# A mixed recurrence, routing and expert kernel on one core: fillers in TensorE's waits, setup constants in the last chunk, and a tile's rows sent to memory by SyncE

## What is computed

```python
# 1: a gated recurrence per batch and head, over t
m_new = max(f_gate[t] + m, i_gate[t])
C = exp(f_gate[t] + m - m_new) * C + exp(i_gate[t] - m_new) * outer(v[t], k[t])
n = exp(f_gate[t] + m - m_new) * n + exp(i_gate[t] - m_new) * k[t]
y[t] = sigmoid(o_gate[t]) * (C @ q[t]) / max(abs(n @ q[t]), 1)
# 2: routing: (token, expert) pairs in falling order of x @ w_gate; a token goes
#    to the first expert that still has room (384 places each)
h = relu(x[mask_e] @ w1[e]);  out[mask_e] = h @ w2[e]          # 320 -> 1024 -> 320
# 3: one more layer pair for all tokens
h = x @ w_in;  g = max(h, 0) + alpha * min(h, 0);  out = g @ w_out   # 320 -> 2048 -> 320
```

## Time and profile before

| | |
|---|---|
| median of 3 runs | 785.16 us (784.6 to 786.09) |
| the profiled execution | 785.32 us, span 783.2 us |
| TensorE products busy | 734.6 us (94%), 5911 instructions |
| VectorE busy | 571.9 us (73%) |
| ScalarE busy | 322.7 us (41%) |
| GpSimd busy | 153.8 us (20%) |
| chain that ended last | PE 85%, DVE 6%, issue 3%, ACT 2%, DMA 1% |

### The profile page before, as it was taken

How to read it: one execution, slowest core, us unless ns; L and a number is a source line. 1 busy time by engine, 2 the same in 40 slices (tenths; PEclk the granted TensorE clock), 3 DMA queues, 4 the chain that set the end, 5 groups by cost and what they waited for, 6 DMA issues and landing times.

```text
span 783.2 us, 17825 instructions
## 1 busy us (share of the span) xinstructions
PE 734.6 (94%) x5911; PEld 689.5 (88%) x5911; DVE 571.9 (73%) x1458; ACT 322.7 (41%) x775; POOL 153.8 (20%) x246
## 2 busy tenths in 40 slices
PE   5999999853999999999999999999999999999994
PEld 4899999742989988998999899889989998999994
DVE  7778888977677868776877778677868777783442
ACT  5666777302234513532361245134413522361431
POOL 6367787401000110110011001101100110011001
PEclk9999999955899999999999999999999999999998
DMA  6888886104104100500320041005001400410000
GB/s 160 251 227 237 224 229 179 42 12 138 42 1 149 31 26 4 175 26 0 88 90 25 0 147 30 25 0 163 31 9 52 125 25 0 142 36 25 1 1 26
DMA packets 66781, 62.54 MB, mean 80 GB/s; under 512 B 35004, under 2 KB 57916, under 8 KB 66748
## 3 DMA queue, kind: packets, MB, share of 16 engines
q1 hardware_dynamic: 57016, 48.66, 21.8%
q0 software_dynamic: 2688, 8.65, 3.5%
q10 hardware_dynamic: 7044, 4.79, 2.0%
HBM read 53.43 MB, written 8.65 MB: 79 GB/s over the span
## 4 chain that ended last, share of the span: by engine, by line
PE 85%; DVE 6%; issue 3%; ACT 2%; DMA 1%; ACTq 1%; POOL 0%; SPq 0%; DVEq 0%
PE bank L924 21%; PE bank L930 18%; PE bank L929 18%; PE bank L948 5%; PE bank L949 4%; PE bank L800 4%; PE bank L783 2%; PE bank L751 2%; PE bank L734 2%; PE bank L974 1%; PE bank L839 1%; PE bank L973 1%; ACT decay L1079 1%; PE bank L848 1%; PE bank L918 1%
## 5 line engine op out<-in xcount | busy, mean ns | idle before, releaser
L924 PE MATMUL bank<-wo_hi,h_hi 128*128 128x320 f32 x384 | 120.6, 314 | 0.0
L930 PE MATMUL bank<-wo_hi,h_lo 128*128 128x320 f32 x384 | 118.6, 309 | 0.0
L929 PE MATMUL bank<-wo_lo,h_hi 128*128 128x320 f32 x384 | 118.0, 307 | 0.0
L1627 DVE SCALAR_TENSOR_TENSOR g_act<-g_neg,rest_alpha,bank 128x384 f32<-128x384 f32 x128 | 78.4, 613 | 40.2 <-ACT g_neg L1161 38.1
L658 POOL DMA_INDIRECT xe<-x_rows,idx_in x24 | 27.0, 1127 | 398.8 <-DVE idx_in L1565 357.7
L1161 ACT ACTIVATE g_neg<-bank 128x384 f32<-128x384 f32 x128 | 62.6, 489 | 94.9 <-PE bank L949 94.9
L1165 ACT CAST h_hi<-g_act 128x384 fp32r<-128x384 f32 x128 | 65.8, 514 | 83.7 <-DVE g_act L1627 83.2
L1159 ACT ACTIVATE h_hi<-bank 128x384 fp32r<-128x384 f32 x64 | 31.5, 492 | 162.3 <-PE bank L949 157.0
L924 PE MATMUL bank<-yT_hi,wi_hi 128*128 128x384 f32 x256 | 92.1, 360 | 0.0
L1632 DVE TENSOR_TENSOR h_lo<-g_act,h_hi 128x384 fp32r<-128x384 f32 x128 | 71.2, 556 | 26.2 <-ACT h_hi L1165 22.5
L929 PE MATMUL bank<-yT_lo,wi_hi 128*128 128x384 f32 x240 | 81.3, 339 | 0.0
(11 more groups left out here) (247 smaller groups left out, 1740.5 us busy)
## 6 DMA issues: line engine op xcount, KB each, us to landing
s<-w SPq DMA_DIRECT2D x8, 1024.0 KB, 5.2
s<-w SPq DMA_DIRECT2D x16, 480.0 KB, 7.2
s<-w SPq DMA_DIRECT2D x16, 256.0 KB, 6.0
k_in<-kT SPq DMA_DIRECT2D x48, 80.0 KB
q_in<-qT SPq DMA_DIRECT2D x48, 80.0 KB
k_row<-k SPq DMA_DIRECT2D x24, 160.0 KB, 3.4
v_in<-v SPq DMA_DIRECT2D x24, 160.0 KB, 3.9
gate_o<-o SPq DMA_DIRECT2D x24, 160.0 KB, 3.3
```

What stands on the lines that cost most here:

```text
L924: pe.matmul(acc, ah, bh, start=start, stop=False, skip_group_check=True)
L929: pe.matmul(acc, ah, bl, start=False, stop=False, skip_group_check=True)
L930: return pe.matmul(acc, al, bh, start=False, stop=stop, skip_group_check=True)
L1627: dve.scalar_tensor_tensor(out=g_act[:, n, :], in0=g_neg[:, :], scalar=rest_alpha[:, j:j + 1], in1=acc, op0=ALU.mult, op1=ALU.add).then_in ...
```

## The change

- `x_sb` and the semaphores `x_out` become four, one for each batch. SyncE writes the rows (`send_rows`): those of tile T - 4 right after it has started `gate_o` of tile T, those of the last four after its last load. VectorE waits also for `x_turned` before it writes a buffer.
- `keep_busy(n, dst)` puts n products of the identity with itself, whose result nobody reads, on TensorE: 14 before the first gates, 5, 2 and 2 in the tail of attention, 12, 3 and 3 before the transposes of the first rows, 2 after them.
- ScalarE's decay waits for `bias_ready`, counted after the first of the three gate copies, not for all three.
- `routing_consts` and `search_consts` move from chunk 0 to chunk 5; `route_tie` counts in `consts`, and VectorE waits for it in `early_bests`.
- `split_peak(1)` runs after the probs of tile 1, not before them.
- w1 comes in slices with a semaphore each (`stage1_in[t]`), and each cast waits for its own; for the first expert ScalarE does `activate(0, 0)` before the second cast of w2.
- In `up`, the first product of the third slice waits for the high part only. In the last `down1` the search's product `add_four` stands one product earlier.

```diff
-        x_sb = ga("x_sb", [P, 2, DM])
+        x_sb = ga("x_sb", [P, B, DM])
...
+            def send_rows(c, b):
+                sp.dma_start(x_rows_by_tile[c, b][:, 0:DM], x_sb[:, b, :]).then_inc(x_out[b], 16)
+                sp.dma_start(x_rows_by_tile[c, b][:, DM:3 * P], x_sb[:, b, 2 * P:DM]).then_inc(x_out[b], 16)
...
                 sp.dma_start(gate_o[:, b, :], o[T]).then_inc(o_in[b], 16)
+                if not first(T, B):
+                    send_rows(c - 1, b)
...
-                sp.dma_start(s1[:, 0:2, :], w1[w, 0:2 * P, :].rearrange("(t p) f -> p t f", p=P)).then_inc(stage1_in, 16)
...
+                for t in range(2):
+                    sp.dma_start(s1[:, t, :], w1[w, P * t:P * t + P, :]).then_inc(stage1_in[t], 16)
...
+            def keep_busy(n, dst):
+
+                for _ in range(n):
+                    pe.matmul(dst[:, 0:P], ident[:, :], ident[:, :], start=True, stop=True)
+
+            keep_busy(14, XTB)
             turn_gates(0)
...
                 if isinstance(T, int) and T >= NT:
+                    keep_busy(5 if T == NT else 2, SCORE[0])
                     pe.wait_ge(out_read, NT)
                     pe.wait_ge(logit_read, T - 2)
                     router(*prev(c, b, 2))
+                if isinstance(T, int) and T == NT:
+                    keep_busy(2, SCORE[0])
...
+                keep_busy(12, UP[2])
                 for m in range(CT):
+                    if m:
+                        keep_busy(3, UP[2])
                     pe.wait_ge(first_rows[m], 16)
...
                 if ready:
+                    pe.wait_ge(ready if highs is None else highs, count + 3)
+                pe.matmul(acc, wh[:, 2, js], ah[:, 2, :], start=False, stop=False, skip_group_check=True)
+                if highs is not None:
                     pe.wait_ge(ready, count + 3)
                 if ready is y_ready:
                     pe.wait_ge(y_twice, count // 3 + 1)
-                pe.matmul(acc, wh[:, 2, js], ah[:, 2, :], start=False, stop=False, skip_group_check=True)
...
                 if b == 0:
-                    act.wait_ge(gates_ready, c + 1)
+                    act.wait_ge(bias_ready, c + 1)
...
-                act.dma_start(x_rows_by_tile[c, b][:, 0:DM], x_sb[:, b % 2, :]).then_inc(x_out[b % 2], 16)
-                act.dma_start(x_rows_by_tile[c, b][:, DM:3 * P], x_sb[:, b % 2, 2 * P:DM]).then_inc(x_out[b % 2], 16)
...
             high_w2(0, 0)
+            activate(0, 0)
             high_w2(0, 1)
-            activate(0, 0)
...
-                if not first(T, 2):
-                    dve.wait_ge(x_out[n], 32 * (c * (B // 2) + b // 2))
+                if not first(T, B):
+                    dve.wait_ge(x_out[b], 32 * c)
+                    dve.wait_ge(x_turned, T - B + 1)
```

More of the change, by code:

```diff
@@ L281, in build_program @@
         gates_ready = sem("gates_ready")
+        bias_ready = sem("bias_ready")
         qk_in = [sem(f"qk_in{b}") for b in range(B)]
@@ L293, in build_program @@
         state_ready = sem("state_ready")
-        x_out = [sem(f"x_out{n}") for n in range(2)]
+        x_out = [sem(f"x_out{b}") for b in range(B)]
         y_done = sem("y_done")
@@ L322, in build_program @@
         token_sum = sem("token_sum")
-        stage1_in = sem("stage1_in")
+        stage1_in = [sem(f"stage1_in{t}") for t in range(3)]
         stage2_in = [sem(f"stage2_in{t}") for t in range(3)]
@@ L483, in _ @@
                 load_tile(NCH - 1, b)
+            for b in range(B):
+                sp.wait_ge(x_ready, NT - B + b + 1)
+                send_rows(NCH - 1, b)
             sp.wait_ge(y_done, NT)
-            for n in range(2):
-                sp.wait_ge(x_out[n], 32 * NT // 2)
+            for b in range(B):
+                sp.wait_ge(x_out[b], 32 * NCH)
             sp.wait_ge(logit_done, NT)
@@ L631, in _ @@
             pool.sem_inc(prep_lo, 4)
-            weigh_values(0, 0)
-            routing_consts()
-            weigh_values(0, 1)
-            search_consts()
-            weigh_values(0, 2)
-            weigh_values(0, 3)
+            for b in range(B):
+                weigh_values(0, b)
             weigh_values(1, 0)
@@ L645, in _ @@
                 if b == 1:
+                    search_consts()
+                if b == 2:
                     mask_consts()
+            routing_consts()
             list_consts()
@@ L675, in _ @@
             pool.sem_inc(out_free, 1)
-            for n in range(2):
-                pool.wait_ge(x_out[n], 32 * NT // 2)
+            for b in range(B):
+                pool.wait_ge(x_out[b], 32 * NCH)
             fetch_rows(0)
@@ L831, in _ @@
             over_chunks(pe, step, tail=(0, 1))
-            pe.wait_ge(consts, 5)
+            pe.wait_ge(consts, 7)
             def count(ph, n):
@@ L919, in turn_rows, with parts3 @@
                 ins.then_inc(xe_turned, 1)
-            def parts3(acc, a, b, start, stop, low=None):
+            def parts3(acc, a, b, start, stop, low=None, between=None):
                 (ah, al), (bh, bl) = a, b
@@ L929, in parts3 @@
                 pe.matmul(acc, ah, bl, start=False, stop=False, skip_group_check=True)
+                if between:
+                    add_four(*between)
                 return pe.matmul(acc, al, bh, start=False, stop=stop, skip_group_check=True)
@@ L970, in down1 @@
                             ins = parts3(ACC[t][:, 0:CAP], (w2_hi[:, j, ds], w2_lo[:, j, ds]),
-                                         (h_hi[:, j % 3, :], h_lo[:, j % 3, :]), j == 0, j == J1 - 1)
+                                         (h_hi[:, j % 3, :], h_lo[:, j % 3, :]), j == 0, j == J1 - 1,
+                                         between=(ph, J1 - 2) if route and j == J1 - 1 and t == 0 else None)
                         else:
@@ L977, in down1 @@
                             ins.then_inc(y_acc, 1)
-                        if route and j == J1 - 1 and t == 0:
-                            add_four(ph, J1 - 2)
                     if route and j == J1 - 1:
@@ L1035, in _ @@
             turn_first()
+            keep_busy(2, UP[2])
             pe.wait_ge(prep_lo, 3 * PREP + 4)
@@ L1254, in copy_gates @@
                     ins = dve.tensor_copy(dst[:, cs, :].rearrange("p c h -> p (c h)"), GATES[i][:, 0:n])
+                    if i == 0:
+                        ins.then_inc(bias_ready, len(GROUPS[g]))
                 ins.then_inc(gates_ready, len(GROUPS[g]))
@@ L1351, in early_bests @@
                 ch = early
+                dve.wait_ge(consts, 7)
                 ch.link(dve.tensor_reduce(row_ones[:, :], ident[:, :].rearrange("p (c r) -> p r c", r=QR), X, ALU.add))
@@ L1412, in make_x @@
                 ch.link(dve.tensor_tensor(scaled[:, :, :], hsum[:, :, 0:D], bc(rnorm[:, :], D), ALU.mult))
-                if not first(T, 2):
-                    dve.wait_ge(x_out[n], 32 * (c * (B // 2) + b // 2))
+                if not first(T, B):
+                    dve.wait_ge(x_out[b], 32 * c)
+                    dve.wait_ge(x_turned, T - B + 1)
                 dve.wait_ge(tanh_ready, T + 1)
-                dve.scalar_tensor_tensor(out=x_sb[:, n, :], in0=gate_o[:, b, :], scalar=1.0, in1=scaled[:, :, :].rearrange("p h d -> p (h d)"),
+                dve.scalar_tensor_tensor(out=x_sb[:, b, :], in0=gate_o[:, b, :], scalar=1.0, in1=scaled[:, :, :].rearrange("p h d -> p (h d)"),
                                          op0=ALU.add, op1=ALU.mult).then_inc(x_ready, 1)
@@ L1424, in step @@
                 if first(T, B):
+                    if b == 0:
+                        split_peak(1)
                     if b == 2:
@@ L1587, in _ @@
             match_rows(ch, 0)
-            dve.wait_ge(consts, 7)
+            dve.wait_ge(consts, 8)
             own_list(ch, 0)
```

14 lines of the change are left out of this document (6 added, 8 removed).

## The result

The changed kernel takes **786.88 us** (785.02 to 788.3) beside 785.16 for the kernel before, run on the same chip: a ratio of 1.0021, 95% interval 1.0013 to 1.0029. It is slower by about 1.7 us; the forecast was 3.6 us faster. The profiled execution took 786.99 us (span 785.2) against 785.32, so it can be read for the difference: +1.67.

A forecast was written before the change was run, and what follows sets the result against it. TensorE was taken as nearly full in attention and experts, with soft places at the start, routing search and first expert's loads. -1.9 + 0.2 + 0 - 0.5 - 1.4 = -3.6 from 785.3 gave 781.7 us; own range 779.5 to 783.6, stated 779.3 to 787.0.

The forecast's parts named there:

- part 2: Attention loop: row writes on SyncE relieve ScalarE, -1.1 us; SyncE's debt costs about 0.2; bounds with the start -3.0, +3.4.
- rival (a): Attention loop: SyncE becomes the bound, 787 to 790 us, chance 0.12; partly bound, near 785.5, another 0.12.
- p = 6.5: SyncE's us a tile in the loop from which the kernel was said to get slower; over 0.2% slower from 6.6.
- p = 6.4: SyncE's us a tile in the loop, between early and later pace; time given as 785.3 + 0.2 = 785.5 us.
- Part 1: First 26 us: fillers raise TensorE's clock, decay waits for the bias first, peak split later; -1.0 us, bounds 0.4 to 1.5.
- Part 3: Last attention chunk: GpSimd's constants moved there collide with VectorE's key chain; +0.2 us, bounds 0 and +1.0.
- Part 4: End of attention: nine fillers in TensorE's waits may hold the clock a few us past 155.75, but VectorE covers it; 0.
- Part 5: Handover to the first expert: earlier casts by slice semaphores, fillers raise the clock; -0.5 us, bounds -1.1 and +0.8.
- Part 6: Hidden-to-output turn of each expert: first product waits for the high part only; 0.17 us eight times, -1.4, bounds -1.8 and -0.6.

The follow-up runs named there:

- k9: Changed kernel with rows issued by ScalarE, with the old start: no fillers before the gates, decay after all three copies, peak split before the second tile; 781.61 us, 0.9953.
- k13: Changed kernel, row writes kept on SyncE, k and q loaded together with two starts a tile in place of four; 780.57 us, 0.9927 of the kernel before.
- k14: Changed kernel with k and q loaded together (two starts in place of four) and the row writes back on ScalarE; 781.47 us, 0.9943 of the kernel before.
- k3: Changed kernel with rows issued by ScalarE and both groups of GpSimd's constants back in chunk 0; 781.08 us, 0.9951 of the kernel before.
- k6: Changed kernel with rows issued by ScalarE, without any of the fillers; 783.4 us, 0.997 of the kernel before.
- k12: Changed kernel with rows issued by ScalarE, one semaphore for all of w1, first activation behind the second cast, fillers kept; 781.81 us, 0.9957 of the kernel before.

## Why the prediction was wrong, by its own steps

**The step that failed is the price of SyncE's tile in part 2, and the slack it was set against.** The price was read off one tile: 4.96 us without waiting, 5.06 with the branch, and 1.1 for the row writes, 6.16 together. The twelve late tiles took 6.43 on average. That one tile was of the kind with wi_raw and wo_raw; every second tile has the two rest_raw starts, which take 0.57 and 0.53 us, not 0.41 and 0.41. Without their row writes the late tiles of the changed kernel take 5.0 us in the first kind and 5.45 in the second. The row writes take 1.12 in a tile like that at 99.81, but in four of the twelve the first of them takes 0.59 to 0.80 instead of 0.36, so they cost 1.2 on average. The four early tiles took 6.98, not 6.6, and the loop began 0.5 us later than the 19.47 counted from.

From there the working of the prediction gives the result: the loads of tile 20 start at 125.08, not 119.8, of which 0.5 lie at the start of the loop, 1.5 in the early tiles and 3.3 in the late ones. The scores start 4.53 later at 129.61 (4.5 was taken), 3.45 after where they stood. This is a sum that fits, not one wait: the trace has the last wait for q at tile 19 (loads 118.81, scores 123.77), and the scores of tile 20 only follow behind it. The other parts bring 1.8 (1.7 was taken), and +3.45 - 1.8 is the +1.67 measured. The 5.3 us between forecast and result are the 5.3 us by which those loads are late.

The prediction had this case twice: as the upper bound of part 2 (+3.4, loads at 125.1, landed at 129.6) and as rival (a), SyncE the bound, at 0.12. It put both wrongly below the forecast. The rival's deciding figure p = 6.5 agrees with the runs (6.57 measured, just slower; 6.02, no loss; 7.39, far slower). Its time for p = 6.4 has a slip: by its own formula that is 0.2 less the 1.7 of the other parts, 783.8 and not 785.5. That 786.9 still lies below the 787.0 at which the stated range ends is no merit of the forecast.

What misled was in the rows. The argument for the low price was that SyncE waits about 1 us a tile late in the loop. Added up, its waits in the kernel before are 9.5 us up to the loads of tile 20, 0.8 for each of the twelve late tiles and none in the four early ones; the other 10.4 us of its waits for x and for TensorE come behind those loads, too late to help. The change adds 1.1 to each of the 16, some 18 us. That alone puts the loads of tile 20 at 113.54 + 18 - 9.5 = 122, an estimate from these numbers, and the forecast of 119.8 out of reach. A second tile would not have shown it: the pair from 77.52 to 89.92 takes 12.40 us with 2.3 of waits, 5.05 a tile, since the start of gate_o takes 0.36 us behind a wait and about 0.5 where SyncE goes straight on.

The Trainium skill ("DMA: Bandwidth & Descriptors", section "Issuing engines are not separate DMA queues") says that transfers started from several engines share the 16 DMA engines and that what is saved is the sequencer's time to start them. The runs agree with it: with the same bytes the kernel takes 781.5 from ScalarE, 786.9 from SyncE and 792.4 from GpSimd, by how full the list of each is; of the last, 4.3 us stand behind the last output copy and have no known cause.

**Part 1, the start: right.** 1.06 at the first value product for 1.0. The fillers took 5.60 us and ended at 8.31 (8.4 was taken), scores took 1.16, VectorE's first probs came at 11.40 (11.35). The experiments don't confirm it in the median (k9). The clock's times in the prediction are a little off: in finer stretches of the kernel before it falls at 155.5, not 155.75, and is back at about 199.88, not 199.56, so 4.6 us after 195.32 and not 4.3.

**Part 2, ScalarE's side: about half.** 0.5 us by the traces of k13 and k14, where 1.1 was taken; TensorE's idle time did go to zero in k13, but part of it goes with the rows on ScalarE too.

**Part 3, the constants: right in the mechanism, small in the sum.** Three operations were longer by 0.3 each, more than one half collision of 0.2, and x of the last tile came 0.6 later against the last value product. Against that the prediction counted no gain for the first chunk, where k3 shows 0.85; the medians show nothing. The Trainium skill ("SBUF — State Buffer", section "Who interferes with whom") says that some VectorE operations, tensor_scalar among them, can take ports that are shared with GpSimd, and that whoever comes first keeps them to the end of its instruction. The three ends 0.1 us behind GpSimd's agree.

**Part 4, the fillers in the tail: right.** The last logits were read at 162.77, 3.93 later, as x of the last tile was. The granted clock stayed at its upper level until about 164.4, where it fell at 155.5 before, and no time came of it.

**Part 5, the first weights: right in kind, small by half.** 1.1 us in place of 0.5. The casts begin at 190.73, 192.26 and 194.51, the first of them 3.7 us earlier against the rest of the program, and the transposes of the rows took 0.55, not 0.90, so the clock had risen before them. The first product came only 0.4 earlier against x of the last tile (+3.56 for +3.93); the rest of the gain lay in the rounds after it, now at full clock. From x of the last tile to the first product of hidden to output it is 45.25 us before, 44.08 in the changed kernel, 44.07 in its twin with the rows on ScalarE, 45.37 without fillers (k6) and 44.78 without the slices (k12). So the gain of 1.2 is gone without the fillers, and over half of it without the slices: the two need each other and can't be added up.

**Part 6, the turns: right.** 1.23 over seven turns, 0.176 each, for 0.17. The two rows that answer to the earlier trace rows:

```profile
372.65 0.34 PE L972 MATMUL bank<-yT_hi,wi_hi 128*128 128x384 f32 x1
373.07 0.44 PE L977 MATMUL bank<-yT_lo,wi_mix 128*128 128x384 f32 x1
```

The high-part product now runs on without a gap, and the wait stands before the low-part one.

## What to carry to other kernels

A queue of transfers is an engine with a pace of its own: before starts are moved to it, add up all that one period of the loop costs it, over every kind of iteration, and set that beside the period of the bound engine. Count a queue's waits as slack only up to the transfer that decides, here 9.5 us against 18 us of added starts. When it is too full, make starts fewer, not smaller: 2 KB starts cost 0.8 to 1.0 us each here, while joining k and q in memory gave back all the time that the moved rows had cost.

## What the runs showed of the hardware

- What a start costs the queue did not follow its size: 160 KB of k_row 0.36 us, a row write of 32 KB 0.35, v_in with 8 pieces a row 0.59, and 2 KB from memory to memory 0.8 to 1.0. From one start to the next it was mostly 0.1 to 0.35 more. Single starts of the same kind sometimes took twice as long or more (k_row 1.62 at tile 6, the first row write 0.80 at tile 13); what delays them is not shown.
- One start of k and q together took about what one of k alone took (two in 0.83 to 0.87 us, against 0.83 to 0.95 for two of k), with twice the bytes.
- The one program with plain row writes in GpSimd's queue (k10_pool_rows) ended 4.3 us later after its last output copy than its twin. No run shows the cause.
